# Attention outputs and their transposes in five chunks of 128 tokens for six of 96, x^T across a bank border

## The reference

```python
# q, k, v: (8 batches, 8 heads, 576 tokens, 64); all fp32
kv  = einsum('bhsd,bhse->bhde', k, v)
o   = einsum('bhsd,bhde->bhse', q, kv)
o   = o / sqrt(mean(o * o, axis=-1) + 1e-6) * g_norm
x   = o.transpose(0, 2, 1, 3).reshape(4608, 512)
x   = (sigmoid(x @ w_gate) * (x @ w_val)) @ w_out        # d_ff 1536
out = (silu(x @ w2_gate) * (x @ w2_val)) @ w2_out
```

## Time and profile before

| | us |
|---|---|
| median of 3 executions | 1740.58 (1739.43 to 1741.91) |
| the profiled execution, whole | 1741.19 |
| its span, first to last instruction | 1738.8 |
| PE busy | 1717.6 (99%) |
| DVE busy | 1204.9 (69%) |
| ACT busy | 890.0 (51%) |
| POOL busy | 376.1 (22%) |

### The profile page before, as it was taken

One profiled execution on the slowest core, in us unless ns is written; L12 is line 12 of the kernel. 1 busy time (PEld: TensorE's weight loads), 2 busy tenths in 40 slices (PEclk: granted clock), 3 DMA queues, 4 the chain that ended last, 5 costly groups with the idle time before them and its releaser, 6 DMA issues.

```text
span 1738.8 us, 30846 instructions
## 1 busy us (share of the span) xinstructions
PE 1717.6 (99%) x11190; PEld 1686.7 (97%) x11190; DVE 1204.9 (69%) x1938; ACT 890.0 (51%) x1709; POOL 376.1 (22%) x326
## 2 busy tenths in 40 slices
PE   8899999999999999999999999999999999999998
PEld 7899999999999999999999999999999999999998
DVE  4876677787666678666679877787666668655556
ACT  5666666555444445444456555555444445444444
POOL 5822222013111125111136000013111124111111
PEclk9999999999999999999999999999999999999999
DMA  9887887586555567555556555576555566555553
GB/s 232 252 264 209 277 254 211 211 298 229 200 200 200 200 222 250 197 198 199 195 188 216 195 198 199 199 250 241 201 198 197 200 220 238 167 180 186 184 187 97
DMA packets 200150, 366.91 MB, mean 211 GB/s; under 512 B 49984, under 2 KB 160064, under 8 KB 200000
## 3 DMA queue, kind: packets, MB, share of 16 engines
q1 hardware_dynamic: 199776, 364.56, 62.8%
q10 hardware_dynamic: 224, 0.39, 0.1%
HBM read 234.36 MB, written 130.55 MB: 210 GB/s over the span
## 4 chain that ended last, share of the span: by engine, by line
PE 93%; DVE 2%; DMA 2%; issue 1%; SPq 0%; POOL 0%; ACT 0%; DVEq 0%; ACTq 0%; POOLq 0%
PE ps L845 87%; PE ps L702 2%; PE ps L687 1%; DMA wops<-in_v_dram 1%; PE ps L692 1%; PE ps L714 1%; PE ps L768 1%; DVE arena L1399 1%; DVE wa L1255 0%; DMA arena<-in_q_dram 0%; DVE arena L1417 0%; DVE xo L1260 0%; PE ps L671 0%; SPq L415 0%; DMA g<-in_g_norm_dram 0%
## 5 line engine op out<-in xcount | busy, mean ns | idle before, releaser
L845 PE MATMUL ps<-xo,wa 128*128 128x384 f32 x6048 | 1076.4, 336 | 4.4 <-DVE arena L1399 1.9
L845 PEld LDWEIGHTS ps<-xo,wa 128*128 128x128 f32 x6048 | 1045.8, 188 | 8.2 <-issue 3.4
L1042 ACT ACTIVATE arena<-ps 128x384 f32<-128x384 f32 x648 | 316.9, 491 | 574.0 <-PE ps L845 572.5
L1399 DVE TENSOR_TENSOR arena<-ps,arena 128x384 f32<-128x384 f32 x648 | 352.3, 553 | 359.0 <-PE ps L845 282.6
L845 PE MATMUL ps<-hop,wb 128*128 128x384 f32 x3024 | 537.9, 335 | 1.2 <-DVE arena L1417 0.9
L845 PEld LDWEIGHTS ps<-hop,wb 128*128 128x128 f32 x3024 | 523.0, 188 | 4.9 <-issue 2.5
L1670 POOL TENSOR_TENSOR arena<-arena 128x384 f32<-128x384 f32 x144 | 146.8, 1045 | 734.9 <-DVE arena L1399 734.9
L1349 DVE TENSOR_TENSOR hop<-arena,hop 128x384 fp32r<-128x384 f32 (+1 forms) x396 | 275.3, 718 | 33.9 <-ACT hop L1024 28.0
L1024 ACT ACTIVATE hop<-arena 128x384 fp32r<-128x384 f32 (+1 forms) x396 | 233.5, 609 | 61.1 <-DVE arena L1417 33.4
L1056 ACT ACTIVATE arena<-arena 128x384 f32<-128x384 f32 x216 | 112.5, 521 | 66.6 <-DVE arena L1399 66.6
L1417 DVE TENSOR_TENSOR arena<-arena 128x384 f32<-128x384 f32 x216 | 129.2, 600 | 20.3 <-DVE arena L1399 1.4
(11 more groups left out here) (75 smaller groups left out, 779.4 us busy)
## 6 DMA issues: line engine op xcount, KB each, us to landing
xo<-x_operands SPq DMA_DIRECT2D x168, 768.0 KB, 6.2
x_operands<-xo SPq DMA_DIRECT2D x84, 768.0 KB, 5.2
x<-arena SPq DMA_DIRECT2D x120, 384.0 KB, 2.9
arena<-x SPq DMA_DIRECT2D x96, 384.0 KB, 4.5
xraw<-x SPq DMA_DIRECT2D x22, 768.0 KB, 6.3
wops<-in_moe_w_gate_dram SPq DMA_DIRECT2D x24, 256.0 KB, 5.1
wops<-in_moe_w_val_dram SPq DMA_DIRECT2D x24, 256.0 KB, 4.5
wops<-in_moe_w_out_dram SPq DMA_DIRECT2D x48, 128.0 KB, 2.3
```

What stands on the lines that cost most here:

```text
L845: mm = pe.matmul(dst, lhsT, rhs, start=(pr in (1, 5, 2) and c == 0 and i == 0), stop=(c == 1 and i == 2), skip_group_check=(pr in (6, 7, 4 ...
L1042: nc.scalar.activation(dst, X(side), ACT.Copy).then_inc(copied, 1)
L1399: nc.vector.tensor_tensor(dst, acc, buf, ALU.add).then_inc(summed, 1)
```

## The change

Outputs are made in five chunks of 128 tokens. 576 is four and a half times 128, so the last chunk starts at token 448 and its first 64 tokens repeat the end of the fourth. The squares, sums, powers and scales run on 128 partitions with 2 x 5 groups of 64 elements. Four transposes then handle 128 tokens each and a fifth takes only partitions 64 to 127 of the last chunk. x^T stands as 576 columns in a row, 512 in one bank and 64 in the next, and is copied out in one pattern. k^T v and q^T stay as they were, with chunks of 96.

```diff
+    OC = -(-S // P)
...
-        ssum = sb("ssum", [SP_, 2, 2 * CH], F32)
+        ssum = sb("ssum", [P, 2, 2 * OC], F32)
...
-        def first_cols(u):
-            return HN if u < UPB else BLK - S
+        def xT_bank(u):
+            return psflat[:, 512 * att_bank(u):512 * att_bank(u) + S]
...
+        psflat = ps[:].rearrange("p b n -> p (b n)")
...
-                for c in range(CH):
+                for c in range(OC):
+                    at = min(c * P, S - P)
                     for h in range(2):
                         hd = slice(h * D, (h + 1) * D)
-                        mm = pe.matmul(ps[0:SP_, att_bank(u) + h, c * D:(c + 1) * D], qT(u)[hd, c * SP_:(c + 1) * SP_],
+                        mm = pe.matmul(ps[:, att_bank(u) + h, c * D:(c + 1) * D], qT(u)[hd, at:at + P],
                                        kv_sb(u)[hd, :], start=True, stop=True)
...
-                lead = first_cols(u) // SP_ if u < SHARED else HALF
-                for c in range(CH):
-                    at = c * SP_ if c < lead else (c - lead) * SP_
-                    mm = pe.transpose(ps[:, att_bank(u) + (c >= lead), at:at + SP_], xn(u)[:, c * P:(c + 1) * P],
-                                      ident[0:SP_, 0:SP_])
+                for c in range(OC):
+
+                    new = slice(0 if c < OC - 1 else OC * P - S, P)
+                    mm = pe.transpose(xT_bank(u)[:, c * P:min((c + 1) * P, S)], xn(u)[new, c * P:(c + 1) * P],
+                                      ident[new, new])
...
-                nc.scalar.activation(dst, ps[0:SP_, b:b + 2, 0:CH * D], ACT.Square).then_inc(squared, 1)
+                nc.scalar.activation(dst, ps[:, b:b + 2, 0:OC * D], ACT.Square).then_inc(squared, 1)
...
-                    dst = xT_place(u)
-                    nc.scalar.activation(dst.rearrange("p (b n) -> p b n", b=2), ps[:, b:b + 2, 0:HALF * SP_],
-                                         ACT.Copy, scale=g2[:]).then_inc(xT_ready, 1)
+                    nc.scalar.activation(xT_place(u), src, ACT.Copy, scale=g2[:]).then_inc(xT_ready, 1)
...
-                    src = ps[0:SP_, b:b + 2, 0:CH * D].rearrange("p h (c d) -> p h c d", d=D)
+                    src = ps[:, b:b + 2, 0:OC * D].rearrange("p h (c d) -> p h c d", d=D)
...
-                r = rrms[:, u % 2].rearrange("p (h c d) -> p h c d", h=2, d=1).to_broadcast([SP_, 2, CH, D])
+                r = rrms[:, u % 2].rearrange("p (h c d) -> p h c d", h=2, d=1).to_broadcast([P, 2, OC, D])
```

More of the change, by code:

```diff
@@ L115, in strassen_mlps @@
         g2 = sb("g2", [P, 1], F32)
-        ssum = sb("ssum", [SP_, 2, 2 * CH], F32)
-        msq = sb("msq", [SP_, 2, 2 * CH], F32)
-        rrms = sb("rrms", [SP_, 2, 2 * CH], F32)
-        mhalf = sb("mhalf", [SP_, 2 * CH], F32)
+        ssum = sb("ssum", [P, 2, 2 * OC], F32)
+        msq = sb("msq", [P, 2, 2 * OC], F32)
+        rrms = sb("rrms", [P, 2, 2 * OC], F32)
+        mhalf = sb("mhalf", [P, 2 * OC], F32)
         taken = [0]
@@ L152, in strassen_mlps @@
         spot[0] = 17 * HN
-        sq_xn = [att(SP_, 2 * CH * D)]
+        sq_xn = [att(P, 2 * CH * D)[:, 0:2 * OC * D]]
         xT_early = [att(P, S)]
-        sq_xn.append(att(SP_, 2 * CH * D))
+        sq_xn.append(att(P, 2 * CH * D)[:, 0:2 * OC * D])
         xT_early.insert(0, att(P, S))
@@ L181, in strassen_mlps @@
         kv_late = att_late(P, D)
-        o_late = [sg.rearrange("p i n -> p (i n)")[0:SP_], att_o[0:SP_]]
+        o_late = [sg.rearrange("p i n -> p (i n)")[:, 0:2 * OC * D], att_o[:, 0:2 * OC * D]]
         def k_in(u):
@@ L931, in unit_sq @@
                         act.wait_ge(xT_made, u - 1)
-                    nc.scalar.activation(xn(u).rearrange("p (c h d) -> p h c d", c=CH, h=2),
-                                         ps[0:SP_, b:b + 2, 0:CH * D].rearrange("p h (c d) -> p h c d", d=D),
+                    nc.scalar.activation(xn(u).rearrange("p (c h d) -> p h c d", c=OC, h=2),
+                                         ps[:, b:b + 2, 0:OC * D].rearrange("p h (c d) -> p h c d", d=D),
                                          ACT.Copy).then_inc(o_taken, 1)
-                    dst = ps[0:SP_, b:b + 2, 0:CH * D]
+                    dst = ps[:, b:b + 2, 0:OC * D]
                 else:
@@ L939, in unit_sq @@
                     dst = sq_xn[u % 2].rearrange("p (h x) -> p h x", h=2)
-                nc.scalar.activation(dst, ps[0:SP_, b:b + 2, 0:CH * D], ACT.Square).then_inc(squared, 1)
+                nc.scalar.activation(dst, ps[:, b:b + 2, 0:OC * D], ACT.Square).then_inc(squared, 1)
             def unit_xT(u):
-                b = att_bank(u)
                 pr = u % UPB
+                src = xT_bank(u)
                 act.wait_ge(xT_made, u + 1)
                 if u < UPB:
-                    nc.scalar.activation(xraw[:, 0, pr, :], ps[:, b, 0:HN], ACT.Copy, scale=g2[:])
-                    nc.scalar.activation(xraw[:, 1, pr, 0:S - HN], ps[:, b + 1, 0:S - HN], ACT.Copy, scale=g2[:]
+                    nc.scalar.activation(xraw[:, 0, pr, :], src[:, 0:HN], ACT.Copy, scale=g2[:])
+                    nc.scalar.activation(xraw[:, 1, pr, 0:S - HN], src[:, HN:S], ACT.Copy, scale=g2[:]
                                          ).then_inc(xT_ready, 1)
                 elif u < SHARED:
-                    nc.scalar.activation(xraw[:, 1, pr, S - HN:HN], ps[:, b, 0:BLK - S], ACT.Copy, scale=g2[:])
+                    nc.scalar.activation(xraw[:, 1, pr, S - HN:HN], src[:, 0:BLK - S], ACT.Copy, scale=g2[:])
                     if u >= UPB + 2:
                         act.wait_ge(xT_stored[u % 2], n_xT(u - 2))
-                    nc.scalar.activation(xT_early[u % 2][:, 0:2 * S - BLK], ps[:, b + 1, 0:2 * S - BLK], ACT.Copy,
+                    nc.scalar.activation(xT_early[u % 2][:, 0:2 * S - BLK], src[:, BLK - S:S], ACT.Copy,
                                          scale=g2[:]).then_inc(xT_ready, 1)
@@ L1280, in unit_scale @@
                 dve.wait_ge(rrms_ready, u + 1)
-                r = rrms[:, u % 2].rearrange("p (h c d) -> p h c d", h=2, d=1).to_broadcast([SP_, 2, CH, D])
-                dst = xn(u).rearrange("p (c h d) -> p h c d", c=CH, h=2)
+                r = rrms[:, u % 2].rearrange("p (h c d) -> p h c d", h=2, d=1).to_broadcast([P, 2, OC, D])
+                dst = xn(u).rearrange("p (c h d) -> p h c d", c=OC, h=2)
                 if u < SHARED:
                     dve.wait_ge(summed_sq, u + 1)
-                    src = ps[0:SP_, b:b + 2, 0:CH * D].rearrange("p h (c d) -> p h c d", d=D)
+                    src = ps[:, b:b + 2, 0:OC * D].rearrange("p h (c d) -> p h c d", d=D)
                 else:
```

## The result

The changed kernel takes 1748.12 us, the median of 5 runs (1747.14 to 1749.57); the kernel before, run beside it, takes 1740.28 (1739.02 to 1741.91). The ratio is 1.0046, its 95% interval 1.0031 to 1.0061. Forecast were 1749.8 us and slower. The profiled execution took 1747.15 us with a span of 1745.4, against 1741.19 and 1738.8.

A forecast was written before the change was run, and what follows sets the result against it. PE, busy 99% of the span, was taken to bound the kernel. Outputs +1.9, x^T +7.3, head +0.5 and shrinking waits -0.5 gave +9.2 us: 1749.8 us, slower by 0.5%, range 1739.5 to 1753.5.

The forecast's parts named there:

- What bounds the kernel: Whole kernel: PE busy 99% of the span; from 79 to 310 us its additions count in full, other engines' savings nothing.
- Part 1, the outputs: L702 block: 24 records of 96 columns become 20 of 128, pair pitch 0.085 becomes 0.112; +0.09 us a unit.
- Rival (b): L702: weight columns don't hold the array, pair pitch stays 0.085; total +3.6 us, 1744.2; chance 0.11.
- Part 2, x^T: L714 block: streamed time unchanged, but the fifth, 64-row transpose changes the array's arrangement; +0.32 us a unit.
- The step that it rests on: PE block borders: passing between 64-partition and full-height arrangements leaves a hole; between two full-height kinds of matmul it doesn't.
- Rival (a): L714: the 64-row transpose changes no arrangement, or leaves no hole; total +1.4 us, 1742.0; chance 0.15.
- (c): L702 and L714: pair pitch stays 0.085 and x^T costs nothing; total -4.5 us, 1736.1, faster; chance 0.07.
- The sum from 79 us on: PE from 79 us on: 21 output blocks add 1.9 us and 23 x^T blocks 7.3 us.
- Part 5: PE's waits for v, 1.0 us in two: a slower PE finds loads landed; -0.5 us.
- Part 3: Other engines: ACT -0.10 us, DVE -0.13 each for sum and scale, POOL's power at best -0.4; zero from 79 us on.
- Part 4, the head: 0 to 79 us: PE's additions against shorter ACT, DVE and POOL chains; +0.5 us, give or take 1.
- Rival (d): x^T ends later against ACT's eviction, so PE newly waits before k^T v; +4 us more, 1754; chance 0.05.

## Why the prediction was right

- *What bounds the kernel.* Right: PE is still busy for 99% and what DVE, ACT and POOL were spared from 79 us on bought nothing: the five full-height chunks have all of it and a ratio of 1.0000.
- *Part 1, the outputs.* Right: +0.09 a unit, measured 0.094; the pitch of 0.112 is there, and the kernel with the outputs alone shows that the stationary columns make it. Rival (b) is out. One comparison beside it was misread: the 160 ns that the prediction derives from the Trainium skill (TensorE: Matmul & The Clock Gate, LDWEIGHTS), columns / 1.2 ns, are for two loads one behind the other. In the trace the two loads of a pair start 7 ns apart and overlap, so the pitch stands against one load, by that formula an estimate of 53, 80 and 107 ns for 64, 96 and 128 columns where the trace has 58, 85 and 112. The page and the trace agree within 5 ns; the sum didn't use it.
- *Part 2, x^T.* Right, and the bulk: +0.32, measured 0.309. Of its terms, entry and first matmul come as 0.20 for 0.11 between the fourth and the fifth start, the exit as 0.20, then 0.28. That is 0.09 in and 0.22 out, where I had 0.15 and 0.17: the total of 0.32 came out better than its parts, and so by some luck. The step that it rests on, that passing between two kinds of matmul of the full height leaves no hole, goes too far: k^T v with 96 rows and 64 stationary columns pays 0.10 on entering as well. The sum is untouched by that, as the change leaves k^T v alone. With 96 rows instead the price is one pitch, with 128 rows in all five it is down to 0.02 a unit. Rival (a) is out, and with it (c), which needed both. The Trainium skill (TensorEngine Tiling (Array Packing), Key Properties) says that a changed tiling mode drains the TensorE; the traces agree, for a transpose as for a matmul, at about 0.3 us for a way out and back.
- *The sum from 79 us on.* 21 x 0.094 + 23 x 0.309 = 9.1, forecast 9.2. In the traces: from unit 9's transposes to the end of the last unit's, from 79.00 to 317.09 before and from 76.82 to 323.14 after, it grows by 246.32 - 238.09 = 8.2 us. The rest of the 9.1 lies in waits that shrank, in part those of Part 5: PE's waits for v are 0.6 us in one where they were 1.0 in two. About 0.6 is a wait that Part 5 didn't name: PE for DVE's sum of a bank, 0.63 us at 92.14 us, which the changed kernel doesn't have.

The wait in the changed kernel's list, then the last unit's transposes, changed and before (PE in order of time; in the latter the run behind them starts 0.44 later, at 317.09):

```profile
PE ps L689 <- DMA wops<-in_v_dram: 0.6, 1, 0.6
```

```profile
322.41 0.80 PE L717 MATMUL ps<-ident,att_o 128*128 128x128 f32 x5
323.14 1.15 PE L848 MATMUL ps<-xo,wa 128*128 128x384 f32 x5
```

```profile
316.65 0.66 PE L714 MATMUL ps<-ident,att_o 96*128 96x96 f32 x6
```

- *Part 3.* ACT -0.10 and DVE -0.13 measured as -0.097 and -0.129. POOL was mis-sized: its power fell by 0.65 us in the mean, 23%, where I allowed a sixth, 0.4. The copy of x^T over the border of two banks takes 738 ns; no price for it shows.
- *Part 4, the head.* The term that failed: +0.5 give or take 1, measured -2.2 at unit 9's transposes. I had put PE's additions there in full and the chain of ACT, DVE and POOL at -0.85 altogether. Other executions agree on the sign: all six profiled heads with five chunks reach unit 9's transposes at 76.39 to 77.79 us, and five of six with six chunks at 78.15 to 79.81 (the sixth, at 86.7, is the one whose clock fell twice). The size is less sure, as the section on the head says: only one of the six with six chunks, before itself, had its clock at 1.00 throughout. That the total is still near the forecast is in part luck, since little or nothing of this term reaches the time.
- *And yet the total.* The head's 2.7 us below forecast isn't all in the time: the median rose by 7.84 us, forecast 9.2. The kernel with the late units alone has none of that head and a ratio of 1.0040 for 1.0046: no gain of the head shows between them, but each interval is over 2 us wide to either side. The spans differ: it grew by 6.6 us in the changed kernel and by 8.1 in that one. How much of the shorter head reaches the end of the changed kernel, between nothing and 1.6 us, stays open.
- *Rival (d).* Out: in steady units no wait of PE for the copy of x^T is left; one of 0.21 us stands at 79.1. ACT ends it at 237.62 + 0.73 = 238.35, 0.45 us before PE takes k^T v at 238.80; I had feared that it would come late, but the gap has grown from 0.15.

ACT in order of time, the changed kernel:

```profile
237.62 0.73 ACT L965 ACTIVATE wops<-ps,g 128x576 f32<-128x576 f32 x1
```

## What to carry to other kernels

Where PE is full, count what an edit does to the array's arrangement before counting instructions or columns: 64 rows, or 64 stationary columns, between blocks of 96 and more cost about 0.1 us on the way in and more on the way out. One small 64-row transpose between full-height matmuls cost 0.3 us, as much as three whole ones of 128 rows, and repeating 64 finished rows was cheaper than skipping them. When the streamed side is short, the loads of the stationary side set the pitch, and then zeros that fill the array (1.04 us) can beat two half-height matmuls (1.27 us). Time won in a head can be handed on to the waits behind it (1.3 of 2.6 us to waits for v, in the kernel whose first units alone were changed): look at those waits before adding it to the sum. And compare heads only between profiles whose clock stood alike there.

## What the hardware showed that I had not expected

The granted clock of PE fell in the head of seven of the twelve profiled runs. In four of them it was from 12 or 14 us on, behind the wait for ACT with which the outputs of units 0 and 1 begin; in three it was elsewhere (20 to 24, 39 to 45 and 63 to 67 us), and the outputs alone had a second fall from 33 to 41. In the kernel before it stood at 1.00. From 12 to 20 us (columns as in the earlier trace rows): changed, and the outputs alone with 128 columns.

```profile
12.00:20.00 8.00, 7.64 (x79) 6.37 (x78) 3.68 (x6) 3.40 (x7) 5.40 (x5) 0.79 1.17 246
```

```profile
12.00:20.00 8.00, 7.99 (x56) 7.05 (x56) 3.34 (x6) 2.87 (x4) 3.44 (x3) 0.57 1.16 252
```

A clock of 1.00 is 2.4 GHz and 0.50 is 1.2 GHz; the values between are stretches with both. In the kernel with the outputs alone it stood at 0.50 from 14 to 18 us, and the outputs of units 0 and 1, 48 records, took 4.86 us there; in the kernel before they took 2.25 at 1.00, and with 128 columns they would take some 2.9 (an estimate: 23 pitches of 0.112 and 0.3 for the last):

```profile
12.01 4.86 PE L703 MATMUL ps<-att_o,arena 64*128 64x64 f32 x48 [0.65 <-ACT att_o L922]
```

```profile
11.90 2.25 PE L702 MATMUL ps<-att_o,arena 64*96 64x64 f32 x48 [0.68 <-ACT att_o L921]
```

PE had waited 0.65 and 0.68 us before them; in the changed kernel it was 0.68 as well, and 0.86 in the kernel with the outputs at full height, whose clock did not fall. So the length of this wait alone doesn't say when the clock falls. In the experiment with the outputs alone the two falls go with a head that is 7.7 us longer. The changed kernel stood at 0.50 from 14 to 16 us, ahead of the long load of q, and still has the shorter head. It falls in timed runs too: their mean granted clocks go from 0.987 to 1.000, and in two runs of the kernel before itself it was 0.993, with 1750.51 and 1751.62 us where the median beside them is 1740.13. That is more than most of these kernels differ by, so a run's clock belongs beside its time.

The second surprise is POOL's power. Its mean is 2847 ns with 12 elements on 96 partitions and 2192 with 10 on 128, more than in proportion; with only the elements changed it is 2505 (10 on 96), and with only the chunks changed 2509 (12 on 128). The shortest ones tell more: 2.26 or 2.27 us for 12 elements and 1.95 for 10, on 96 or 128 partitions alike. So the elements make about 0.3 us of the 0.65, and the other half isn't in the power's own size; it comes where the chunks are of 128, most likely by what runs beside it.
